# Sparse attention, MLP and routed experts on one core: where small TensorE jobs stand in a hand-written order of places

## The reference

```
k_sum = k.reshape(B,H,24,32,D).max(axis=3);  v_sum = v.reshape(B,H,24,32,D).mean(axis=3)
scores = [masked(scale*q@k.T, |i-j|<16), scale*q@k_sum.T + log(32)]
x = softmax(scores) @ [v, v_sum]              # -> 1536 tokens x 512
x = elu(x @ w_in) @ w_out                     # 512 -> 2048 -> 512
logits = (x/|x|) @ (emb/|emb|).T / tau        # 8 experts
e = argmax(logits); gate = softmax(logits)[e]
out = gate * (relu(x @ w1[e]) @ w2[e])        # 512 -> 1024 -> 512, the chosen expert of each token
```

## Time and profile before

| | |
|---|---|
| median of 3 runs | 526.49 us (525.84 to 526.74) |
| the profiled execution | 526.66 us |
| its span, first to last instruction | 524.9 us |
| PE busy | 511.5 us, 97% of the span |
| DVE, ACT, POOL busy | 332.2, 213.2, 92.5 us |
| granted clock of PE | 0.999 |

### The profile page before, as it was taken

One profiled execution on the slowest core, in us unless ns is written; L12 is line 12 of the kernel. 1 busy time (PEld: TensorE's weight loads), 2 busy tenths in 40 slices (PEclk: granted clock), 3 DMA queues, 4 the chain that ended last, 5 costly groups with the idle time before them and its releaser, 6 DMA issues.

```text
span 524.9 us, 11573 instructions
## 1 busy us (share of the span) xinstructions
PE 511.5 (97%) x3754; PEld 439.7 (84%) x3755; DVE 332.2 (63%) x712; ACT 213.2 (41%) x480; POOL 92.5 (18%) x223
## 2 busy tenths in 40 slices
PE   8799999999999999999999999999999999999994
PEld 7588888888888888888898999887788888888883
DVE  3679899687867665767554568767573473222662
ACT  5668654433443334333432445441531441111440
POOL 6412121002340000000000001002221211111221
PEclk9999999999999999999999999999999999999999
DMA  8899415586445335332412710102964155101000
GB/s 193 259 340 314 89 35 117 133 150 122 105 117 109 66 66 138 74 61 51 120 42 61 301 41 18 33 33 72 353 225 168 40 183 191 40 29 37 20 20 25
DMA packets 125899, 60.24 MB, mean 115 GB/s; under 512 B 95382, under 2 KB 113814, under 8 KB 125856
## 3 DMA queue, kind: packets, MB, share of 16 engines
q1 hardware_dynamic: 123456, 53.38, 37.4%
q0 software_dynamic: 2400, 6.30, 3.6%
HBM read 50.22 MB, written 11.01 MB: 117 GB/s over the span
## 4 chain that ended last, share of the span: by engine, by line
PE 94%; SPq 2%; DMA 1%; issue 1%; ACT 1%; DVE 0%; POOLq 0%; DVEq 0%; ACTq 0%
PE bank L1051 26%; PE bank L1095 9%; PE bank L1102 9%; PE bank L1108 8%; PE bank L1258 5%; PE bank L1304 5%; PE bank L1266 5%; PE bank L1312 5%; PE bank L1260 5%; PE bank L1306 5%; PE bank L1029 3%; PE bank L1296 2%; PE bank L999 2%; DMA v_raw<-in_v 1%; PE bank L1163 1%
## 5 line engine op out<-in xcount | busy, mean ns | idle before, releaser
L1459 ACT ACTIVATE el<-bank 128x512 f32<-128x512 f32 x48 | 28.6, 597 | 98.4 <-PE bank L1051 98.1
L1051 PE MATMUL bank<-x_hi,w_hi_parts 128*128 128x256 f32 x376 | 60.8, 284 | 0.0
L1051 PE MATMUL bank<-x_lo,w_hi_parts 128*128 128x256 f32 x376 | 60.1, 282 | 0.0
L1051 PE MATMUL bank<-x_hi,w_lo_parts 128*128 128x256 f32 x376 | 60.0, 282 | 0.0
L1051 PEld LDWEIGHTS bank<-x_hi,w_hi_parts 128*128 128x128 f32 x376 | 53.4, 188 | 3.7 <-issue 0.2
L1783 DVE TENSOR_SCALAR el<-el 128x512 f32<-128x512 f32 x48 | 20.6, 429 | 55.0 <-ACT el L1459 55.0
L1095 PE MATMUL bank<-w_hi_parts,g_hi 128*128 128x512 f32 x192 | 54.9, 407 | 0.0
L1102 PE MATMUL bank<-w_lo_parts,g_hi 128*128 128x512 f32 x192 | 52.7, 396 | 0.0
L1108 PE MATMUL bank<-w_hi_parts,g_lo 128*128 128x512 f32 x192 | 52.2, 393 | 0.0
L789 POOL COPY kb<-kT 128x96 f32<-128x96 f32 x96 | 26.2, 316 | 143.7 <-PE bank L999 123.3
L1051 PEld LDWEIGHTS bank<-x_lo,w_hi_parts 128*128 128x128 f32 x376 | 51.3, 188 | 0.0
(11 more groups left out here) (292 smaller groups left out, 871.6 us busy)
## 6 DMA issues: line engine op xcount, KB each, us to landing
raw<-in_moe_w SPq DMA_DIRECT2D x8, 2048.0 KB, 8.9
w_raw<-in_moe_w_in SPq DMA_DIRECT2D x8, 512.0 KB, 6.4
w_raw<-in_moe_w_out SPq DMA_DIRECT2D x8, 512.0 KB, 6.5
p_rows<-p_all SPq DMA_DIRECT2D x16, 256.0 KB, 2.4
p_squares<-p_rows SPq DMA_DIRECT2D x64, 64.0 KB, 2.4
v_raw<-in_v SPq DMA_DIRECT2D x8, 384.0 KB, 4.5
x_rows<-x SPq DMA_DIRECT2D x6, 512.0 KB, 3.2
x<-x_rows SPq DMA_DIRECT2D x20, 128.0 KB, 2.8
```

The source lines that it names most:

```text
L1051: mm = pe.matmul(o, r32(w[:, at:at + P]), r32(x[i % 2][:, c, :]), start=(part == "hh" and c == 0), stop=(part == "lh" and c == DC - 1))
L1459: act.activation(el[n % 2], bank[:, H_BANK[n % 2], :], ACT.Exp).then_inc(e_act, 1)
```

## The change

Means of batch 1 move by two places, from 21, 25, 29, 33 to 23, 27, 31, 35, and from the scores' bank to `T_BANK`. In exchange for the waits with `stt` and `made` they are turns of kind 0 in `T_TURNS`. The dots of blocks 0 to 3 move by one place, from offset 10 to 11; the ranks of blocks 0 to 3 by three, from 12 to 15; those of block 4 stay. Everything of EMB_AT moves by two places, so the embeddings' transposes stand at 19 instead of 17. In PE's `between` the means now come first, then embeddings, values and scores, and dots and ranks come last. On ACT the means' copy comes ahead of `store_x_high`; on DVE dots and ranks come behind `softmax_max`.

All the new places hold values and scores too, but for two: place 75 (dots of block 3) holds values alone, and place 79 (ranks of block 3) holds no other PE job. At 79 DVE also has `norms(0)` and `shifted_logits(0)`.

```diff
-    M_PLACES = (21, 25, 29, 33)
+    M_PLACES = (23, 27, 31, 35)
...
     def d_at(i):
-        return PER_BLOCK * (i + 1) + 10
+        return PER_BLOCK * (i + 1) + (11 if i < NB - 2 else 10)
     def k_at(i):
-        return PER_BLOCK * (i + 1) + 12
+        return PER_BLOCK * (i + 1) + (15 if i < NB - 2 else 12)
...
-    EMB_AT = PER_BLOCK - 4
+    EMB_AT = PER_BLOCK - 2
...
-    T_TURNS = sorted([(d_at(i), 1, i) for i in range(NB - 1)]
+    T_TURNS = sorted([(d_at(i), 1, i) for i in range(NB - 1)] + [(M_PLACES[g], 0, g) for g in range(PAIRS)]
...
             def means(g):
                 pe.wait_ge(rows_ok, 1)
                 pe.wait_ge(v_sum, g + 1)
-                pe.wait_ge(vs_ev, PAIRS + g)
-                pe.wait_ge(stt, sum(s_at(u) < M_PLACES[g] for u in UNIT_RANGE if u >= PAIRS))
+                t_bank_free(M_PLACES[g], 0)
...
-                mm = pe.matmul(bank[KW:KC, S_BANK[0], 0:P], mean_rows[0:V_ROWS, :], rows[:, :, 0, :],
+                mm = pe.matmul(bank[KW:KC, T_BANK, 0:P], mean_rows[0:V_ROWS, :], rows[:, :, 0, :],
...
+                    if kind == 0:
+                        pe.wait_ge(vs_ev, PAIRS + n + 1)
...
-                made = sum(m < s_at(u) for m in M_PLACES)
-                if made > 0:
-                    pe.wait_ge(vs_ev, PAIRS + made)
...
             def between(place):
+                for g in range(PAIRS):
+                    if M_PLACES[g] == place:
+                        means(g)
                 if place == EMB_AT + 5:
                     t_bank_free(place, 5)
                     transpose_embeddings()
...
-                for g in range(PAIRS):
-                    if M_PLACES[g] == place:
-                        means(g)
+                for i in range(NB - 1):
+                    if d_at(i) == place:
+                        t_bank_free(place, 1)
+                        route_dots(i, T_BANK)
+                    if k_at(i) == place:
+                        t_bank_free(place, 3)
+                        ranks(i, T_BANK)
...
                 act.wait_ge(m_mm, PAIRS + g + 1)
                 act.wait_ge(o_mm, (BPB - 1) * PAIRS + g + 1)
                 act.copy(vwin[KW:KC, g, :, :],
-                         bank[KW:KC, S_BANK[0]:S_BANK[0] + 1, 0:P].to_broadcast([NSUM, WINS, P])
+                         bank[KW:KC, T_BANK:T_BANK + 1, 0:P].to_broadcast([NSUM, WINS, P])
```

More of the change, by code:

```diff
@@ L936, in t_bank_free @@
                     _, kind, n = T_TURNS[at - 1]
-                    pe.wait_ge({1: l_ev, 2: pT_ev, 3: rank_v, 4: list_ok, 5: emb_enT}[kind], n + 1)
+                    if kind == 0:
+                        pe.wait_ge(vs_ev, PAIRS + n + 1)
+                    else:
+                        pe.wait_ge({1: l_ev, 2: pT_ev, 3: rank_v, 4: list_ok, 5: emb_enT}[kind], n + 1)
             def o_bank_free(place, kind):
@@ L1519, in behind @@
                     shifted_exps(0)
+                for g in range(PAIRS):
+                    if M_PLACES[g] == place:
+                        evacuate_means(g)
                 for u in range(PAIRS, BY_SQUARES):
@@ L1528, in behind @@
                         evacuate_p(u)
-                for g in range(PAIRS):
-                    if M_PLACES[g] == place:
-                        evacuate_means(g)
             def exps_behind(place):
@@ L1939, in behind @@
                         turn_x2(i)
[L1940 to L1948, removed]
                 for u in STEADY:
@@ L1977, in behind @@
                         softmax_max(u)
+                for i in range(NB - 1):
+                    if d_at(i) == place:
+                        store_dots(i, T_BANK)
+                        experts(i)
+                    if k_at(i) == place:
+                        store_ranks(i, T_BANK)
+                        if i == STAR_BLOCK:
+                            choose_first()
+                        if i == LIST_BLOCK - 1:
+                            leave_gap()
                 for g in range(PAIRS):
```

## The result

The changed kernel takes 524.33 us (median of 6 runs, 523.96 to 524.98), the kernel before 526.16 us in the same comparison (6 runs, 525.61 to 526.74). The ratio is 0.9965, 95% interval [0.9953, 0.9978]. Two further comparisons with more runs gave 0.9985 [0.9976, 0.9993] and 0.9978 [0.9969, 0.9987]; the kernel before against itself gave 0.9998 [0.9988, 1.0007] and 1.0006 [0.9998, 1.0015]. So it is faster, by 0.24% as the mean of the three, 1.3 us and not the 2.0 of the forecast. The profiled execution took 524.4 us, its span is 522.7 us, the granted clock 0.998.

The account below looks back on a forecast made before the run. PE's issue of matmuls was taken as the bound; means 0.84, embeddings 0.21, dots 0.92 and ranks 0 sum to 1.97 us, taking the median 526.49 to 524.5 us, range 523.9 to 525.6.

Parts of the forecast that it names:

- The borders of the means (0.84): PE: four means joined to values and scores each save 0.21 us of slowed neighbouring groups, 0.84 us together.
- the embeddings (0.21): PE: the embeddings' transposes, moved to an already interrupted place, save the same border as the means, 0.21 us.
- the dots (0.92): PE: four dots, joined to values and scores or values alone, each save a border of 0.23 us, 0.92 together.
- the 0.43: PE: sign against the forecast, if means ahead of values stand this many us or more; 0.33 was expected.
- Ranks 0, with bounds of plus and minus 0.10: PE: moving the ranks behind the scores saves nothing, within 0.10 us either way for each of three.
- The cover check: ACT, DVE, SP and POOL: whether they still deliver in time for PE after the moves; no stall counted, 0.2 us at worst.
- Yardsticks that stay as they are: PE: uninterrupted groups keep their old distances, such as 1.39 us over two groups, so they add nothing to the sum.
- the forecast margin of 0.2: PE at 27 and 31: ACT's copy of the means frees `T_BANK` 0.2 us before dots or ranks are due.
- half of the borders: Rival: means ahead of values or dots behind scores keep a slow start of 0.10 us each; 525.6 us, chance 0.10.
- margin was used up: Rival: PE stalls at 27, 31 and 79 as cover runs out, up to 0.8 us; 525.2 us, chance 0.06.
- ACT at place 18: Rival: squares hold ACT so long that `project(11)` waits for `g_hi(11)`; about 527.6 us if 6 us more, chance 0.04.
- the first rival: PE: half of the borders stay, so nine joined jobs save only 0.9 us; 525.6 us, chance 0.10.

Follow-up runs that it names:

- the probes: changed kernel plus eight extra unread means products, alone at eight places or four each at two places ahead of values: 528.70 us alone, 526.38 us joined.
- `ranks_ahead`: changed kernel with the ranks put ahead of the values, dots and means still between values and scores: 524.04 us in a single run.
- `dots_only`: kernel before with only the dots moved, and dots and ranks last within a place on PE and DVE: 527.36 us in a single run.
- `ranks_back`: changed kernel with only the ranks put back at their old offset 12: 526.41 us.
- The ten waits: changed kernel with the scores' old, always fulfilled waits on `made` put back in PE's queue: 524.41 us in a single run.
- `probes_joined`: changed kernel with eight extra unread means products, four each at places 51 and 55 ahead of the values: 526.38 us.

## Why the prediction was right, and what it missed

- **The borders of the means (0.84), the embeddings (0.21) and the dots (0.92): right.** The places gave 1.85 us against 1.97, and 1.73, 2.17 and 1.96 each against 1.71, 2.15 and 1.94; the probes gave the same price. What is missing is mostly the dots: alone at 42 and 58 they had cost 0.76 and not the 0.79 of place 26. The means stand 0.33 us ahead of the values, well under the 0.43 that would have spoken against the forecast, and no row of PE from 94 to 120 us names a releaser. The rule of the Trainium skill, TensorEngine Tiling (Array Packing), Key Properties, is that changing the tiling mode drains the engine. The trace agrees: 0.09 us behind a small job, even between two small shapes.
- **"Ranks 0, with bounds of plus and minus 0.10": right, as the sum of two costs that cancel.** Joined they add 0.44 to 0.47 us to a place, alone they cost 0.44 to 0.46. Their own part grew by 0.11 (0.13 against 0.03 us to the second record), which the prediction feared for their weight loads, and about as much fell away at their borders. `ranks_ahead` shows that the 0.11 goes with standing behind the scores; that it is a weight load that finds nothing to hide behind is a reading and not shown. Not in the sum at all: the ranks of block 4 keep their place, but the new order within a place puts them behind the transposes, and their own part grew by 0.08, of which the transposes gave 0.06 back.
- **What the ranks' move is for: missed.** I costed the edits one by one and gave the ranks "0", as if the dots could move without them. `dots_only` and `ranks_back` show that DVE's `oh_r` is then late three times, for 1.3 to 1.8 us of waits. The cover check asked what the new DVE order delays on `g_low`, and not who waits for the dots' own result.
- **Yardsticks that stay as they are: the step that failed.** The sum took every uninterrupted group at its time before. The plain groups rose by 0.8 us in all, and this one term, which the sum held at nothing, is as large as the means' whole gain. The cause is open. The ten waits and the order of the ranks are excluded. Their excess is 0.19 to 0.23 us in the kernel before, 0.32 with the means joined, 0.56 with the dots, 0.71 with means, dots and embeddings and 1.00 with all; but it isn't the number of joined jobs alone, since four means add 0.1 and four dots 0.35, and the eight further products of `probes_joined` leave it at 1.02.
- **The cover: right.** At place 27 ACT's copy ended at 126.41 and the dots started at 126.61, the forecast margin of 0.2. At 79 `g_lo` was done at 300.90 for a reader at 301.28, margin 0.38 against 0.3. At place 18 `el(11)` started at 100.74 and `g_hi(11)` ended at 103.16; with the 1.67 us by which this execution began earlier that is 102.4 and 104.8, forecast 102.3 and 105. ACT and DVE, kernel after:

```profile
100.74 0.58 ACT L1458 ACTIVATE el<-bank 128x512 f32<-128x512 f32 x1
102.54 0.62 ACT L1464 CAST g_hi<-el 128x512 fp32r<-128x512 f32 x1 [0.96 <-DVE el L1784]
...
125.83 0.58 ACT L1409 COPY vwin<-bank 24x512 f32<-24x512 f32 x1
```

```profile
300.21 0.69 DVE L1789 TENSOR_TENSOR g_lo<-el,g_hi 128x512 fp32r<-128x512 f32 x1
```

- **The predicted 524.5 us** agrees with 524.33, and partly by luck: 1.97 forecast less 1.0 that didn't come, made up in the profiled executions of the first comparison by a start 1.67 us earlier, less 0.42 behind it. The three comparisons together, 0.24%, lie near the bound of what can be told from no change, not well behind it.
- **The rivals.** No half of the borders stayed, no margin was used up, ACT at place 18 was in time. The stretch's 1.0 us resembles the first rival's 0.9 in size, by another mechanism that none of the four named.

## What to carry to other kernels

A small job between two long ones on PE pays for its borders, here 0.2 us a job, and pays them once when several stand together; look for places that are interrupted already. Before a producer is moved, check its consumer: the dots needed the ranks to move with them, since DVE lies between. And read a gain of this size from a stretch between two matmuls, which repeated to 0.05 us here, and not from the span, whose start alone wandered by 0.8 us within one kernel with the landing of one load.

## What was not expected of the hardware

- PE's uninterrupted matmuls have more than one rhythm at the same granted clock (0.996 to 0.999). The 36 matmuls of a step take 5.627, 5.638, 5.662 or 5.67 us. In the fastest a project group of four stands 0.922 to 0.936 us from the next and a hidden group 0.467 to 0.479; in the slowest 0.930 to 0.934 and 0.477 to 0.483. The kernel before keeps the fastest in 12 of 13 such steps. In the kernel after the level also changes from one step to the next with no job between, and each came out the same to 1 ns in all three executions.
- A change between two small array shapes costs 0.09 us, as much as one between a small shape and the whole array. With the whole array behind it, the next long group is slower by 0.10 us as well.
- A full-array matmul of 16 columns lets the next follow after 0.03 us behind long matmuls, after 0.13 behind the scores' short ones, after 0.11 behind four transposes and after 0.10 when PE had stood idle.
